# Two-layer dense product behind a decayed linear attention: an opening whose loads come in the order of need, a first dense product in halves, and the last two up products of the second layer in a row

## The reference

```python
def _attn_ref(q, k, v):                     # B, H, S, D = 4, 8, 768, 64
    for t in range(S):
        state = gamma[None, :, None, None] * state + np.einsum('bhd,bhe->bhde', k[:, :, t], v[:, :, t])
        y[:, :, t] = scale * np.einsum('bhd,bhde->bhe', q[:, :, t], state)

def _moe_ref(x, w_in, w_out):               # 3072 tokens, 512 -> 2048 -> 512
    h = x @ w_in
    g = np.where(h >= 1, h, np.where(h <= -1, 0.0, (h + 1) ** 2 / 4))
    return g @ w_out

def _moe2_ref(x, w_in, w_out, g_ln):        # 512 -> 1024 -> 512
    h = x @ w_in
    solu = h * softmax(h)
    ln = (solu - mean(solu)) / np.sqrt(var(solu) + 1e-06) * g_ln
    return ln @ w_out
```

## Time and profile before

| what | value |
|---|---|
| runs shown | 885.4 us median of 3 (884.4 to 888.78) |
| profiled execution's own time | 884.47 us |
| span of its trace, first to last instruction | 882.6 us |
| busy: PE, DVE, ACT, POOL | 868.1, 401.7, 282.8, 204.8 us |

### The profile page before, as it was taken

One profiled execution on the slowest core, in us unless ns is written; L12 is line 12 of the kernel. 1 busy time (PEld: TensorE's weight loads), 2 busy tenths in 40 slices (PEclk: granted clock), 3 DMA queues, 4 the chain that ended last, 5 costly groups with the idle time before them and its releaser, 6 DMA issues.

```text
span 882.6 us, 11875 instructions
## 1 busy us (share of the span) xinstructions
PE 868.1 (98%) x4864; PEld 710.8 (81%) x4864; DVE 401.7 (46%) x645; ACT 282.8 (32%) x438; POOL 204.8 (23%) x185
## 2 busy tenths in 40 slices
PE   6999999999999999999999999999999999999997
PEld 5788888888888888888878888888888888888886
DVE  4444443333433243333433333443666666666662
ACT  2333342122212132221321232334344444444432
POOL 2555433223222323222212122226000000000000
PEclk9999999999999999999999999999999999999999
DMA  9912102111111112211111004300444444444442
GB/s 347 344 49 71 62 12 86 48 48 48 51 58 48 48 36 80 64 49 37 48 36 48 25 1 167 120 1 0 144 136 159 148 143 143 155 144 162 148 139 100
DMA packets 50741, 82.83 MB, mean 94 GB/s; under 512 B 5248, under 2 KB 23680, under 8 KB 50688
## 3 DMA queue, kind: packets, MB, share of 16 engines
q1 hardware_dynamic: 50400, 81.56, 27.3%
q10 hardware_dynamic: 288, 0.53, 0.2%
HBM read 56.90 MB, written 25.17 MB: 93 GB/s over the span
## 4 chain that ended last, share of the span: by engine, by line
PE 96%; DMA 1%; SPq 1%; DVE 0%; ACT 0%; issue 0%; DVEq 0%
PE acc L360 31%; PE h L347 29%; PE o_ps L731 15%; PE h L716 15%; PE att L281 2%; PE att L292 2%; PE att L316 1%; DMA mask<-in_mask 1%; PE att L306 1%; SPq L194 1%; SPq L211 0%; SPq L212 0%; ACT w L387 0%; DVE w L511 0%; ACT g_raw L436 0%
## 5 line engine op out<-in xcount | busy, mean ns | idle before, releaser
L360 PE MATMUL acc<-g_hi,w 128*128 128x512 f32 x768 | 257.1, 396 | 0.0
L347 PE MATMUL h<-x_hi,w 128*128 128x512 f32 x768 | 252.3, 389 | 3.2 <-DVE x_lo L476 2.1
L624 POOL TENSOR_TENSOR g_lo<-g_raw,g_hi 128x512 fp32r<-128x512 f32 x96 | 123.4, 1286 | 403.0 <-ACT g_hi L387 403.0
L436 ACT ACTIVATE g_raw<-g_raw,half_bias 128x512 f32<-128x512 f32 x96 | 69.6, 724 | 341.9 <-DVE g_raw L560 341.9
L360 PEld LDWEIGHTS acc<-g_hi,w 128*128 128x128 f32 x768 | 144.1, 188 | 35.1 <-issue 3.4
L347 PEld LDWEIGHTS h<-x_hi,w 128*128 128x128 f32 x768 | 144.1, 188 | 33.5 <-ACT x_hi L387 2.4
L360 PE MATMUL acc<-g_lo,w 128*128 128x512 f32 x384 | 149.6, 390 | 0.0
L347 PE MATMUL h<-x_lo,w 128*128 128x512 f32 x384 | 149.4, 389 | 0.0
L560 DVE TENSOR_SCALAR g_raw<-h 128x512 f32<-128x512 f32 x96 | 66.2, 690 | 178.5 <-PE acc L360 177.8
L565 DVE TENSOR_TENSOR g_raw<-h,g_raw 128x512 f32<-128x512 f32 x96 | 66.4, 692 | 70.0 <-ACT g_raw L436 70.0
L347 PEld LDWEIGHTS h<-x_lo,w 128*128 128x128 f32 x384 | 72.1, 188 | 14.9
(11 more groups left out here) (68 smaller groups left out, 814.5 us busy)
## 6 DMA issues: line engine op xcount, KB each, us to landing
z<-zq SPq DMA_DIRECT2D x24, 512.0 KB, 2.6
zt<-z SPq DMA_DIRECT2D x96, 128.0 KB, 2.9
kT<-in_kT SPq DMA_DIRECT2D x24, 256.0 KB, 2.6
q<-in_q SPq DMA_DIRECT2D x24, 256.0 KB, 2.7
v<-in_v SPq DMA_DIRECT2D x24, 256.0 KB, 3.0
x2T<-y SPq DMA_DIRECT2D x24, 256.0 KB, 2.5
x_raw<-x2T SPq DMA_DIRECT2D x12, 512.0 KB, 4.4
out<-o SPq DMA_DIRECT2D x24, 256.0 KB, 2.0
```

The costliest lines, as they stand in the source:

```text
L347: last = mm(hb[f % 2][:, :], ww, xx[:, kt, :], start=kt == 0 and t == 0, stop=kt == KT - 1 and t == 2)
L360: last = mm(acc[m][:, :], ww, gg[:, f % 2, :], start=f == 0 and t == 0, stop=f == FT1 - 1 and t == 2)
L436: nc.scalar.activation(gate[:, f % 2, :], gate[:, f % 2, :], ACT.Square, bias=half_bias[:, 0:1], scale=0.5).then_inc(sem["squared"], 1)
L624: tt(g[1][:, f % 2, :], gate[:, f % 2, :], g[0][:, f % 2, :].bitcast(F32), ALU.subtract)\
```

## The change

1. **Loads by need.** `first_mask` moves from ACT's queue into SP's, third behind kT0 and q0; v0 and v1 come between the chunks' kT and q; w_in and w_out are loaded apart: w_in runs three pieces ahead (`W_READY` = 3), w_out(0) comes behind the four kn.
2. **Splits apart.** w_in and w_out of a piece have an ACT copy each (`split_w_in`, `split_w_out`); w_out(f) is split in the step f that it belongs to, on ACT behind g_hi(f) and on POOL behind g_lo(f), no longer two steps ahead.
3. **Opening of TensorE.** Three products of a zeroed tile run first (`WARM_UP`); `outputs(c)` comes behind `scores(c + 2)`, no longer behind all scores; the first dense product, `first_up`, is made in two halves of 256 columns, each of which waits for two chunks only; POOL makes the lo part of w_in(0).
4. **States later.** The four updates move from slots 0 to 3 to slots 2 to 5 (`FIRST_UPDATE` = 2). DVE's waits for `mask` and `tables` move to their first users.
5. **End.** The last up product comes ahead of down(19), right behind up(22); DVE's, ACT's and SP's last two tiles are interleaved accordingly.

```diff
-W_READY = 2
+W_READY = 3
+WARM_UP = 3
+FIRST_UPDATE = 2
...
             for c in range(B):
                 load("kT", c)
                 load("q", c)
-            for c in range(2):
-                load("v", c)
-            load_weights(0)
+                if c == 0:
+                    sp.dma_start(mem["first_mask"][:, :, :, :].rearrange("p e a t -> p (e a t)"), io["first_mask"])\
+                        .then_inc(sem["first_mask"], 16)
+                if c >= 2:
+                    load("v", c - 2)
+            load_w_in(0)
             for c in range(2, B):
                 load("v", c)
-            load_weights(1)
+            for f in range(1, W_READY):
+                load_w_in(f)
             sp.dma_start(tables[:, :], io["tables"]).then_inc(sem["tables"], 16)
             for c in range(B):
                 load("kn", c)
-            load_weights(2)
+                if c == 1:
+                    load_w_in(W_READY)
+            load_w_out(0)
+            load_w_in(W_READY + 1)
+            load_w_out(1)
...
+            def first_up():
+                for b in (0, 2):
+                    xs = slice(b * P, (b + 2) * P)
+                    pe.wait_ge(sem["x0_hi"], b + 2)
+                    if b == 0:
+                        pe.wait_ge(sem["w_in_hi"], 1)
+                    for t, (wn, xn) in enumerate(((0, 0), (1, 0), (0, 1))):
+                        if t == 1:
+                            pe.wait_ge(sem["w0_in_lo"], 1)
+                        if t == 2:
+                            pe.wait_ge(sem["x0_lo"], b + 2)
+                        for kt in range(KT):
+                            last = mm(hb[0][:, xs], w[0][:, wn, kt * P:(kt + 1) * P], x[xn][:, kt, xs],
+                                      start=t == 0 and kt == 0, stop=t == 2 and kt == KT - 1)
+                last.then_inc(sem["h_ready"], 1)
...
+            pe.wait_ge(sem["warm"], 1)
+            for n in range(WARM_UP):
+                mm(acc[KT - 1][:, 0:2 * P], mem["warm"][:, 0:P], mem["warm"][:, :], start=True, stop=True)
+            scores(0)
+            scores(1)
             for c in range(B):
-                scores(c)
-            for c in range(B):
+                if c + 2 < B:
+                    scores(c + 2)
                 outputs(c)
...
-            for c in range(B - 1):
+            first_split(0)
+            split_w_in(0)
+            for c in range(1, B):
                 first_split(c)
...
-            for f in range(W_READY):
-                split_weights(f)
+            pool.wait_ge(sem["w_in_hi"], 1)
+            tt(w[0][:, 1, :], w_raw[0][:, 1, :], w[0][:, 0, :].bitcast(F32), ALU.subtract)\
+                .then_inc(sem["w0_in_lo"], 1)
...
-                if t >= LAG2:
+                if LAG2 <= t < TILES - 2:
                     down(t - LAG2)
-            for t in range(TILES - LAG2, TILES):
+            for t in range(TILES - 2 - LAG2, TILES):
                 down(t)
...
+            maximum(TILES - 2)
+            softened(TILES - 2)
+            maximum(TILES - 1)
+            normalized(TILES - 2)
+            softened(TILES - 1)
+            split_z(TILES - 3)
+            normalized(TILES - 1)
+            split_z(TILES - 2)
             split_z(TILES - 1)
```

More of the change, by code:

```diff
@@ L93, in place @@
     plain("half_bias", [P, 1])
-    plain("warm", [P, 1])
+    plain("scratch", [P, 1])
+    plain("warm", [P, BLK // 2])
     for name in STATISTICS:
@@ L235, in _ @@
             load_chunk(B)
-            for f in range(3, FIRST_PIECE):
-                load_weights(f)
+            for f in range(2, FIRST_PIECE):
+                if f + W_READY < FIRST_PIECE:
+                    load_w_in(f + W_READY)
+                load_w_out(f)
             sp.wait_ge(sem["probs"], 2 * B)
@@ L328, in attention @@
             def attention(j, slot):
-                if j == 1 and slot < B:
-                    update(slot)
+                if j == 1 and 0 <= slot - FIRST_UPDATE < B:
+                    update(slot - FIRST_UPDATE)
                 for c, stage in at_slot(j, slot, STAGES):
@@ L365, in dense @@
                 for f in range(FT1):
-                    up(blk, f)
+                    if blk == 0 and f == 0:
+                        first_up()
+                    else:
+                        up(blk, f)
                     if blk < BLOCKS - 1:
@@ L439, in dense @@
                     copy(g[0][:, f % 2, :], gate[:, f % 2, :]).then_inc(sem["g_hi"], 1)
[L440 to L441 removed]
+                    if blk == 0:
+                        if f + W_READY < FT1:
+                            split_w_in(f + W_READY)
+                        split_w_out(f)
                     if blk == BLOCKS - 1:
                         prepare(f)
[L445 to L446 removed]
             act.dma_start(mem["g_ln"][:, :], io["g_ln_col"]).then_inc(sem["gains"], 16)
             act.wait_ge(sem["half_set"], 1)
[L449 to L450 removed]
+            nc.scalar.activation(mem["scratch"][:, :], half_bias[:, :], ACT.Copy)
+            first_split(0)
+            split_w_in(0)
+            for c in range(1, B):
                 first_split(c)
[L452 to L453 removed]
             for f in range(1, W_READY):
[L455 removed]
+                split_w_in(f)
             for blk in range(BLOCKS):
@@ L481, in take_outputs @@
                 dve.wait_ge(sem["y_ready"], c + 1)
+                if c == B:
+                    dve.wait_ge(sem["tables"], 16)
                 if b == 0:
@@ L569, in dense @@
                         prepare(f)
+            nc.vector.memset(mem["warm"][:, :], 0.0).then_inc(sem["warm"], 1)
             nc.vector.memset(half_bias[:, :], 0.5).then_inc(sem["half_set"], 1)
@@ L574, in _ @@
                 mask_scores(c)
-            for c in range(B - 1):
+            for c in range(B):
                 first_split(c)
-            split_weights(0)
-            first_split(B - 1)
             for f in range(1, W_READY):
                 split_weights(f)
-            dve.wait_ge(sem["tables"], 16)
-            dve.wait_ge(sem["mask_loaded"], 16)
             dve.wait_ge(sem["gains"], 16)
@@ L764, in output, with exponential @@
                 copy(o[:, t % 2, :], op[t % 2][:, :]).then_inc(sem["o_ready"], 1)
-            for t in range(TILES):
-                if t >= 2 and t % 2 == 0 and t // 2 + 1 < TILES // 2:
-                    split_x(t // 2 + 1)
+            def exponential(t):
                 act.wait_ge(sem["neg_max"], t + 1)
@@ L775, in _ @@
                                      accum_out=st("sq_sum", t)).then_inc(sem["sq_sum"], 1)
+            for t in range(TILES - 2):
+                if t >= 2 and t % 2 == 0 and t // 2 + 1 < TILES // 2:
+                    split_x(t // 2 + 1)
+                exponential(t)
+                squares(t)
                 if t == 0:
@@ L781, in _ @@
                     split_z(t - 1)
-            output(TILES - 3)
+            exponential(TILES - 2)
+            squares(TILES - 2)
+            exponential(TILES - 1)
+            split_z(TILES - 3)
+            squares(TILES - 1)
+            output(TILES - 5)
+            split_z(TILES - 2)
+            output(TILES - 4)
             split_z(TILES - 1)
-            output(TILES - 2)
-            output(TILES - 1)
+            for t in range(TILES - 3, TILES):
+                output(t)
         @block.vector
@@ L802, in split_z, with maximum @@
                         .then_inc(sem["zT_lo"], 1)
[L804 to L808, removed]
+            def maximum(t):
                 dve.wait_ge(sem["h2_ready"], 2 * t + 2)
-                nc.vector.tensor_reduce(st("h_max", t), h, AX.X, ALU.max).then_inc(sem["h_max"], 1)
+                nc.vector.tensor_reduce(st("h_max", t), hp[t % 2][:, :], AX.X, ALU.max).then_inc(sem["h_max"], 1)
                 dve.wait_ge(sem["h_max"], t + 1)
@@ L837, in _ @@
                     .then_inc(sem["zq_ready"], 1)
+            dve.wait_ge(sem["power_set"], 1)
+            for t in range(TILES - 2):
+                if t >= 2 and t % 2 == 0 and t // 2 + 1 < TILES // 2:
+                    split_x(t // 2 + 1)
+                maximum(t)
+                softened(t)
+                if t == 0:
+                    finish["dve_evacuate"]()
+                normalized(t)
                 if t:
                     split_z(t - 1)
+            maximum(TILES - 2)
[3 more added lines that the diff above has]
+            softened(TILES - 1)
+            split_z(TILES - 3)
+            normalized(TILES - 1)
+            split_z(TILES - 2)
             split_z(TILES - 1)
```

44 lines of the change are left out of this document (24 added, 20 removed).

## The result

The changed kernel takes 881.45 us (median of 9 runs, 878.71 to 882.18) against 885.14 for the kernel before (9 runs, 884.06 to 888.78). The ratio is 0.9949 [0.9933, 0.9964]: faster, by 0.51% in the middle of an interval from 0.36 to 0.67%, so on the edge of the 0.5% that the prediction names as the least that can be told. The forecast was 878.0, the range up to 881.5, which holds the median by 0.05 us. The gain has the right sign and a little over half of the forecast size (3.7 us instead of 7.0).

The account below looks back on a forecast made before the run. PE was taken as the bound, busy 868.1 of 882.6 us, with only the opening and end open. Gains of 5.2 and 1.8 us sum to 7.0, from the runs' median to 878.4, forecast 878.0; range 876.0 to 881.5.

Parts of the forecast that it names:

- The end: Last up and down products: tile 23 is ready in time and PE's wait of 1.5 us goes; gain 1.8 us.
- The halves: First dense product: 24 passes of 256 columns at 0.115 us, costed at nothing; upper end 4.5 us.
- PE without a wait from the first dense product to the block edge: From first_up at about 14.8 us PE runs to down(0) at 25.3, and is full from there.
- signs of being wrong: scores(2) over 1.5 us; PE waiting over half a microsecond for x_lo, kn or w_out; zT_lo releasing down(22) or down(23).
- With first_mask as two units of 256 KB: Opening loads: first_mask counted as two units in the load order, landing at 6.0 us, q1 at 7.4.
- landing rule: Opening loads: unit n of 256 KB lands at 3.35 + 0.67 n us, 1.85 us later from `tables` on.
- the pauses of the new order are shorter: Opening of PE: pauses shorter than the 2.14 us wait behind which passes went at full clock before.
- The rival of the low clock: Opening: low clock lasts through scores(2), first_up starts 1.5 us later, 879.5 us; chance 0.15.
- Its counter-argument: Against the low clock in the opening: clock rose some 4.7 us after first scores before; warm-up only adds work.
- Two ACT copies for one: some 0.2 us a step in block 0: Separate w_in and w_out copies on ACT, an engine a third busy; listed under what costs nothing.
- later steps have more room: Behind down(0): w_out(f) is ready about 2.4 us later behind g_lo(f), and steps after the first have more slack.
- The slower rival: Clock stays low in dense products from first_up to down(0), some 2.4 us lost each, five give 890.0; chance 0.05.

Follow-up runs that it names:

- run 7: Changed kernel with six more zeroed products behind scores(0), and the first dense product whole, 12 passes of 512 columns: 881.85 us, ratio 0.9969.
- Run 3: Changed kernel with the first_mask load alone put back on ACT's queue: 880.25 us, ratio 0.9949.
- run 1: Kernel before with part 5 of the change (the end) and nothing else: 882.7 us against 884.75, ratio 0.9978.
- run 2: Changed kernel with six more products of the zeroed tile behind scores(0), to keep TensorE busy: 879.57 us, ratio 0.9943.
- run 8: Changed kernel with six more zeroed products behind scores(0) and the split of w_out(14) one step earlier: 878.95 us, ratio 0.9934.
- run 5: Changed kernel with first_mask on ACT's queue, w_out(14) split one step earlier and five warm-up products instead of three: 878.34 us, ratio 0.9927.
- run 4: Changed kernel with the split of w_out(14) one step earlier, on ACT and POOL: 880.86 us, ratio 0.9953.
- run 9: Changed kernel with first_mask two places later in SP's queue, behind kT1 and q1, and w_out(14) split one step earlier: 878.85 us, ratio 0.993.
- run 6: Changed kernel without the three warm-up products: 881.3 us, ratio 0.9961.
- run 10: Changed kernel with first_mask on ACT's queue, w_out(14) split one step earlier and no warm-up products: 879.33 us against 884.63, ratio 0.9933.

## Why the prediction was half right

**What held.** The end: 1.8 forecast, 2.05 measured alone. The halves: at 3.07 us for 24 passes, restart included, they are far from the bound, if a little over the 2.9 that the prediction named, and run 7 shows that they save 0.7 us or more. PE without a wait from the first dense product to the block edge: in the changed kernel 28.64 - 18.19 = 10.45 us lie between first_up and down(0), forecast 25.3 - 14.8 = 10.5. The sign follows from these.

**Where it failed.** That the median lies inside the range, by 0.05 us, is luck: the upper end was drawn for rivals of which one came, and the late loads and the block edge had no part in it. Two of the signs of being wrong that the prediction names did come: scores(2) took 1.94 us, and PE waited 0.51 us for x_lo. Three steps failed, all before 14.8 us or in a place costed at nothing:

- *"With first_mask as two units of 256 KB"*: the landing rule came from a stretch in which two queues were loading, `first_mask` on ACT's. In SP's queue it landed some 2.8 us behind q0, about twice two units, though the loads behind it were moving meanwhile. q1 landed at 8.36, forecast 7.4, and the loads behind it, up to v3, about a microsecond late. Run 3 (the same order, the mask on ACT) has q3 at the forecast 10.7.
- *"the pauses of the new order are shorter"* than 2.14 us, behind which the clock had stayed up. The forecast had one of 0.6 us ahead of scores(1), from 6.9 to 7.5. It was 2.96: 1.0 more because of the step above, and 1.4 more because scores(0) was done at 5.54. The prediction had put scores(0) at the low clock, 4.8 to 6.9, and so left out what its own warm-up does. Even with q1 on time the pause would have been 1.9 us. Behind 2.14 the clock fell as well in run 1. The rival of the low clock had 0.15 and a price of 1.5 us; it came, and cost 2.4: from scores(1) to first_up passed 18.19 - 8.50 = 9.69 us where the forecast had 14.8 - 7.5 = 7.3. Its counter-argument, that the warm-up only adds work, overlooked that work done before a pause does not help behind it. The Trainium skill's warning (TensorE: Matmul & The Clock Gate, Part 1) that idling brings the low clock back, quoted there against this change, agrees with 0.50 from 8.50 to 14.10.
- *"Two ACT copies for one: some 0.2 us a step in block 0"*, put under what costs nothing, and *"later steps have more room"*: true in the other steps of block 0, where PE waits for none of these. In the step that also splits x the new copy and POOL's subtraction lie on PE's path. By the trace 0.8 us, by runs 2 and 8 0.6.

**The account.** Mending these one by one goes from 881.45 to the forecast: the clock 1.9 (to 879.57, run 2; with the proviso on medians made there), the block edge 0.6 (to 878.95, run 8), the loads 0.6 (to 878.34, run 5), against 878.0. These are differences of medians whose ratio intervals overlap, so each size is less sure than the trace behind it. In run 5 the opening still gains 4.78 us instead of 5.2, read at the second down product. What is left there are restarts: 12 passes behind one of the scattered updates take 2.94 us, elsewhere 2.72, and in the new order updates lie between products at three places, before at two. The prediction read the groups as 2.72 us throughout and took 2.8 for an up product, though the trace of before has 2.95 behind other work (37.88 above). Grouping the updates was not tried.

**The slower rival** (0.05), half clock in the dense products, did not come in the changed kernel: the clock is back at 14.6, before first_up. Run 1 shows that its first condition is met at times, dense passes at half clock behind a pause; that five products in a row were slow was seen in no run.

## What to carry to other kernels

Price a warm-up and the first wait behind it together: zeroed products are worth something only if TensorE stays busy until real work follows, so look where the load after next lands before adding them. A landing rule read where two queues were loading need not hold where the large load stands in the one queue; leave such a load beside the queue rather than in it, or behind what is needed first. When work is moved into "its own" step, look for the one step of the loop that already has extra work.

## What the hardware showed that was not expected

- **The same length of pause did and did not cost the clock.** Behind 2.14 us of idling the dense passes ran at full pace in the profile of before and at 0.50 in run 1; 2.32 us cost it (run 4), 2.52 did not (run 9), 2.96 did. The length alone does not decide here. The Trainium skill, TensorE: Matmul & The Clock Gate, Part 1, says that the number of slow matmuls at a start differs from run to run of one kernel; the spread of 3.5 us of the changed kernel fits that, but run 7, kept busy, spreads over 2.6, so it is not shown here.
- **The column of granted clock can be wrong at the start.** Before, it reads 1.00 from 0 us on the earlier trace rows, while scores(0) takes 2.08 us, the pace of 1.2 GHz; likewise in run 3 for the scores at 6.06. The pace of a known pass is the better witness there.
- **With `first_mask` in SP's queue less is moved.** From 6 to 7 us it was 250 GB/s in the changed kernel and between 285 and 387 in runs 2, 4, 6, 7 and 8, which have the same order, so it differs between executions; with the load on ACT's queue it was between 395 and 410 (before and runs 1, 3, 5 and 10). What limits it is open.
- **Two engines' subtractions hold each other up.** Each of x_lo's four takes 0.68 us undisturbed. In run 8 the longest, beside g_lo on POOL, takes 1.37; in the changed kernel the second, beside w_out's, takes 1.78, and POOL's own 1.74, where run 8 has 1.28. Instructions of x_lo, after and run 8 (shortest, median and longest in ns):

```profile
L562 DVE TENSOR_TENSOR x_lo<-y,x_hi x4: 677/761/1778, 116.4 to 119.5; 128x512 fp32r<-128x512 f32 x4
```

```profile
L565 DVE TENSOR_TENSOR x_lo<-y,x_hi x4: 677/678/1369, 113.1 to 115.6; 128x512 fp32r<-128x512 f32 x4
```

The Trainium skill, SBUF — State Buffer, section SBUF: two separate sides, says that DVE with two SBUF inputs and GpSimd take turns at one pair of ports; the rows agree: the one that waits is longer by 0.5 to 1.1 us, less than the other's whole subtraction. The prediction's 1.75 us for one of POOL's, half of 3.49, has such waiting in it; w_in(0)'s took 1.28 in the changed kernel.
